# Banded attention by two steps at a time, with one output bank and two banks for turned probabilities

## The reference

```python
scores = scale * np.matmul(q, k.transpose(0, 1, 3, 2))
rel = pos[:, None] - pos[None, :]
is_global = pos[None, :] < int(n_global)            # n_global = 8
is_local = (rel >= 0) & (rel < int(n_local))        # n_local = 96
keep = is_global | is_local
dist = np.where(is_global & ~is_local, float(n_local), np.abs(rel))
scores = scores - slopes[:, None, None] * dist      # slopes by head
scores = np.where(keep, scores, -1e9)
a = softmax(scores); out = np.matmul(a, v)
```

## Time and profile before

| | us |
|---|---|
| median of 3 runs | 1066.98 (1065.27 to 1067.94) |
| profiled execution | 1066.19 |
| its span | 1064.5 |
| PE busy | 944.0 (89%) |
| DVE busy | 691.9 (65%) |
| ACT busy | 443.8 (42%) |
| granted PE clock, mean | 0.923 of full |

### The profile page before, as it was taken

One profiled execution on the slowest core, in us unless ns is written; L12 is line 12 of the kernel. 1 busy time (PEld: TensorE's weight loads), 2 busy tenths in 40 slices (PEclk: granted clock), 3 DMA queues, 4 the chain that ended last, 5 costly groups with the idle time before them and its releaser, 6 DMA issues.

```text
span 1064.5 us, 22298 instructions
## 1 busy us (share of the span) xinstructions
PE 944.0 (89%) x6394; PEld 772.3 (73%) x6397; DVE 691.9 (65%) x1855; ACT 443.8 (42%) x950; POOL 187.8 (18%) x247
## 2 busy tenths in 40 slices
PE   6999999977699999999999993444599999999994
PEld 4667777665488888888888883333388989898984
DVE  5787887758775869878787775555545544464521
ACT  3777777744553534525525251000033434252410
POOL 1222222300111111111111110000113122321211
PEclk8999999989799999999999997555699999999997
DMA  9677676533171515334333342000134444535100
GB/s 212 133 154 143 143 148 147 119 128 143 26 271 39 197 49 197 126 120 178 127 139 119 128 149 97 2 2 2 31 109 155 172 157 169 197 128 195 52 30 30
DMA packets 146569, 129.41 MB, mean 122 GB/s; under 512 B 102464, under 2 KB 114752, under 8 KB 146368
## 3 DMA queue, kind: packets, MB, share of 16 engines
q1 hardware_dynamic: 137696, 99.68, 31.8%
q0 software_dynamic: 8800, 28.84, 8.0%
HBM read 107.79 MB, written 20.71 MB: 121 GB/s over the span
## 4 chain that ended last, share of the span: by engine, by line
PE 78%; DVE 9%; issue 5%; SPq 2%; DVEq 2%; ACT 1%; DMA 1%; ACTq 0%; POOL 0%; POOLq 0%
PE ps_o L1272 14%; PE ps_s L1249 14%; PE ps_o L1614 8%; PE ps_s L1598 6%; PE ps_pT L1598 6%; PE ps_s L1614 4%; PE ps_pT L483 4%; PE ps_o L501 4%; PE ps_s L470 3%; PE ps_t L1775 3%; PE ps_pT L1260 2%; PE ps_t L455 1%; PE ps_o L510 1%; PE ps_t L1235 1%; DVE arena_p L689 1%
## 5 line engine op out<-in xcount | busy, mean ns | idle before, releaser
L1272 PE MATMUL ps_o<-w_split_parts,hs 128*128 x696 | 168.7, 398 | 7.5 <-issue 7.5
L1249 PE MATMUL ps_s<-w_split_parts,xs 128*128 x696 | 165.5, 393 | 1.0 <-ACT xs L1341 1.0
L1272 PEld LDWEIGHTS ps_o<-w_split_parts,hs 128*128 128x128 f32 x696 | 130.0, 190 | 34.9 <-issue 8.0
L1459 DVE SCALAR_TENSOR_TENSOR product<-y_sb,wg_all 128x512 bf16<-128x512 f32 x224 | 145.8, 688 | 10.7 <-issue 5.2
L1249 PEld LDWEIGHTS ps_s<-w_split_parts,xs 128*128 128x128 f32 x696 | 128.6, 188 | 26.6 <-issue 1.3
L1614 PE MATMUL ps_o<-w_split_parts,hs 128*128 128x512 f32 x384 | 94.4, 397 | 0.0
L800 ACT ACTIVATE arena_p<-arena_p,min_s 128x256 f32<-128x256 f32 (+1 forms) x192 | 91.9, 485 | 5.1 <-DVE min_s L678 5.1
L1450 DVE TENSOR_TENSOR w_split_parts<-raw,w_split_parts 128x1024 f32 (+1 forms) x68 | 78.8, 1220 | 19.2 <-ACT w_split_parts L1360 17.8
L1614 PEld LDWEIGHTS ps_o<-w_split_parts,hs 128*128 128x128 f32 x384 | 70.2, 188 | 16.2 <-ACT hs L1648 2.9
L1694 DVE TENSOR_TENSOR w_split_parts<-raw,w_split_parts 128x1024 fp32r<-128x1024 f32 x56 | 68.6, 1224 | 18.3 <-ACT w_split_parts L1656 18.1
L678 DVE CUSTOM_DVE_ANT_0 arena_p<-ps_s,arena_b 128x256 f32<-128x256 f32 (+1 forms) x144 | 53.8, 392 | 39.7 <-PE ps_s L470 16.9
(11 more groups left out here) (307 smaller groups left out, 1653.1 us busy)
## 6 DMA issues: line engine op xcount, KB each, us to landing
raw<-in_moe_w SPq DMA_DIRECT2D x32, 2048.0 KB, 9.1
y_rows<-y_sb POOLq DMA_DIRECT2D x31, 256.0 KB, 2.4
kn<-in_k SPq DMA_DIRECT2D x32, 192.0 KB, 3.5
qn<-in_q SPq DMA_DIRECT2D x32, 192.0 KB, 3.8
vn<-in_v SPq DMA_DIRECT2D x32, 192.0 KB, 3.2
x_rows<-arena_x SPq DMA_DIRECT2D x96, 64.0 KB, 1.6
va<-in_v SPq DMA_DIRECT2D x32, 120.0 KB, 3.1
wg_rows<-in_moe_w_gate SPq DMA_DIRECT2D x1, 2048.0 KB, 8.1
```

The source lines that it names most:

```text
L1249: last = nc.tensor.matmul(ps_s[:, f, :], xs[:, a, c * P:(c + 1) * P], weights(par, w, cols), start=(n == 0), stop=(n == len(passes) - 1))
L1272: last = nc.tensor.matmul(ps_o[:, 0, :], hs[:, a, c * P:(c + 1) * P], weights(par, 2 + w, slice(c * DM, (c + 1) * DM)), start=(n == 0), st ...
L1459: nc.vector.scalar_tensor_tensor(product[:, e % 2, :], y_sb[:], 1.0, wg_all[:, e, :], ALU.mult, ALU.mult, accum_out=log_now[:, e:e + 1])
```

## The change

Steps are taken in twos. `two_pairs` runs over t = 0 to 5, and two-step t has the steps 2t and 2t + 1.
- Scores: both steps of a two-step are scored in one group, into two banks of 512 columns (256 for each step), and the two pairs of banks take turns. The fourth score bank is now `ps_o[:, 1]`, so that `ps_o[:, 0]` is the one output bank; the freed `ps_pT[:, 1]` makes a second bank for turned probabilities.
- Turned probabilities and value products of both steps are issued in groups.
- `copy_cols`, `turn_back` and `norm` run every two steps, over 256 columns; adding and inverting the sums is a function of its own, `invert`.
- Four steps can be held, not three. Steps 3, 7, 9 and 11 are kept by ACT.
- The turns are placed one in each two-step (all three in round 0 of the first pass), and ACT's and DVE's parts of a group stand in the same two-step as the turn; `splits_of` is gone.
- ACT's exps go one two-step ahead of the turned probabilities: in round t it does those of steps 2t + 2 and 2t + 3, which are biased in the same round.
- Counts of semaphores are adapted, in the dense form too, which doesn't run with these inputs.

The core of the diff:

```diff
-        KEPT_BY_ACT = (2, 4, 8, 10)
+        TWOS = QT
+        KEPT_BY_ACT = (3, 7, 9, 11)
         def turns_of(first, last_one):
+            if last_one:
+                return {0: [(0, 2)]}
+            return {0: [(0, 0), (0, 1), (0, 2)] if first else [(0, 2)], 1: [(1, 0)], 2: [(1, 1)], 3: [(1, 2)], 4: [(2, 0)], 5: [(2, 1)]}
...
             def two_pairs(it, first, last_one):          # PE
+                for t in range(TWOS):
+                    if t + 1 < TWOS or not last_one:
+                        score(it, t + 1)
+                    if t >= 2:
+                        turn_back(it, t - 2)
+                    elif not first:
+                        turn_back(it - 1, t - 2 + TWOS)
+                    turn_probs(it, t)
+                    for nth, g in turns_of(first, last_one).get(t, ()):
                         turn(it * 2 + nth + 1, it + (nth + 1) // 2, (nth + 1) % 2, g)
+                    if t >= 1:
+                        value(it, t - 1)
+                    elif not first:
+                        value(it - 1, TWOS - 1)
...
             def value(it, t):
+                pe.wait_ge(normed, it * 6 + t + NORM0)
...
+            def invert(it, t):                           # DVE
+                s = sums_b[:, 4 * t:4 * t + 4]
+                dve.wait_ge(exped, it * 24 + 4 * t + 4 + ATT0)
                 nc.vector.tensor_scalar(s, s, 1e-9, None, ALU.add)
                 dve.drain()
                 nc.vector.reciprocal(s, s)
                 dve.drain()
...
             def two_pairs(it, first, last_one):          # DVE
+                for t in range(TWOS):
+                    before_it, back = (it, t - 2) if t >= 2 else (it - 1, t - 2 + TWOS)
+                    done_one = t >= 2 or not first
+                    if done_one:
+                        invert(before_it, back)
+                    if t + 1 < TWOS or not last_one:
+                        bias_scores(it, 2 * t + 2)
+                    if done_one:
+                        norm(before_it, back)
+                    if t + 1 < TWOS or not last_one:
+                        bias_scores(it, 2 * t + 3)
+                    for s in (2 * t, 2 * t + 1):
+                        if s not in KEPT_BY_ACT:
+                            keep_turned(it, s)
+                    for nth, g in turns_of(first, last_one).get(t, ()):
                         low_qk(it * 2 + nth + 1, (nth + 1) % 2, g)
...
             def two_pairs(it, first, last_one):          # ACT
+                for t in range(TWOS):
+                    if t + 1 < TWOS or not last_one:
+                        exp(it, 2 * t + 2)
+                    for s in (2 * t, 2 * t + 1):
+                        if s in KEPT_BY_ACT:
+                            keep_turned(it, s)
+                    if t + 1 < TWOS or not last_one:
+                        exp(it, 2 * t + 3)
+                    for nth, g in turns_of(first, last_one).get(t, ()):
                         high_qk(it * 2 + nth + 1, (nth + 1) % 2, g)
+                    if t >= 1:
+                        copy_cols(it, t - 1)
+                    elif not first:
+                        copy_cols(it - 1, TWOS - 1)
```

More of the change, by code:

```diff
@@ L456, in turn @@
                 last.then_inc(qk_turned, 1)
[L458 to L466, removed]
-                    for hh in range(2):
[L468 to L488, removed]
-                    pe.wait_ge(v_in[par], it * 96 + 96)
[L491 to L504, removed]
@@ L511, in turn_back @@
+            def turn_back(it, t):
+                pe.wait_ge(o_copied, it * 6 + t + 1)
+                for j in range(2):
+                    last = nc.tensor.transpose(ps_o[:, 0, j * P:(j + 1) * P], o_cols[:, j * P:(j + 1) * P], ident[:])
                 last.then_inc(o_turned, 1)
             def two_pairs(it, first, last_one):
[L514 to L519, removed]
-                    elif not first:
[L521 to L528, removed]
+                for t in range(TWOS):
[3 more added lines that the diff above has]
+                        turn_back(it, t - 2)
+                    elif not first:
+                        turn_back(it - 1, t - 2 + TWOS)
+                    turn_probs(it, t)
+                    for nth, g in turns_of(first, last_one).get(t, ()):
@@ L535, in pe_banded @@
                 turn(0, 0, 0, g)
-            for s in range(AHEAD):
-                score(0, s)
+            score(0, 0)
             two_pairs(0, True, False)
@@ L712, in two_pairs @@
                         low_qk(it * 2 + nth + 1, (nth + 1) % 2, g)
-                    if s % 3 == 2 and s > 2:
-                        norm(it, s // 3 - 1)
-                    elif s == 2 and not first:
-                        norm(it - 1, 3)
                 if last_one:
-                    norm(it, 3)
+                    for t in (TWOS - 2, TWOS - 1):
+                        invert(it, t)
+                        norm(it, t)
             for g in range(3):
                 low_qk(0, 0, g)
-            for s in range(AHEAD):
+            for s in range(2):
@@ L818, in two_pairs, with copy_cols @@
[L818 to L828 removed]
+            def copy_cols(it, t):
+                act.wait_ge(valued, it * 24 + 4 * t + 4 + ATT0)
+                if not (isinstance(it, int) and it == 0 and t == 0):
+                    act.wait_ge(o_turned, it * 6 + t)
+                nc.scalar.activation(o_cols[:], ps_o[:, 0, 0:2 * P], ACT.Copy).then_inc(o_copied, 1)
```

147 lines of the change are left out of this document (79 added, 68 removed).

## The result

| | before | changed |
|---|---|---|
| median of the runs, us | 1067.46 (1065.27 to 1068.86, 4 runs) | 1102.62 (1102.12 to 1103.87, 4 runs) |
| ratio, 95% interval | | 1.0333 [1.0313, 1.0353] |
| span of the profiled execution, us | 1064.5 | 1100.4 |
| mean granted clock | 0.923 | 0.915 |
| one pass of the attention loop, us | 25.5 | 30.9 |

The change makes the kernel 35 us slower, 3.3%. The attention alone ends 36.7 us later (263.26 - 226.53), so next to nothing is lost behind it. The forecast was 1080, slower, with the range 1065 to 1096: the sign and the mechanism are right, the size is not.

A forecast was written before the change was run, and what follows sets the result against it. It took a DVE to ACT to DVE loop each round to bound attention: start 2.4, six passes 165.6, further rounds 22.6 and 19.2 sum to 209.8 against 196.5, +13.3 on 1066.2 us: 1079.5, say 1080; range 1065 to 1096.

The forecast's parts named there:

- which loop decides: Banded attention: a DVE to ACT to DVE loop once a round makes a pass 27.6 us, 2.1 more than before.
- PE, the output bank and the keeps hide in it: Attention rounds: PE's 3.5 us fit in 4.6; one output bank's cost and DVE's keeps are covered by the loop.
- PE alone: TensorE in an attention pass: 26 fewer shape changes by 0.17 us save 4.4, leaving 21.1 us if nothing makes it wait.
- the new norm: DVE's 256-column norm, absent from the trace, priced like the 256-column copy: 0.42 less 0.08 overlap, 0.34 us.
- Base 1.64 + 0.46 + 0.98 + 0.03 = 3.11: Loop length before high and low parts, in us: DVE to second biases, bias to exp, two exps, release of DVE.
- the 0.61 within the 1.64: DVE's add, reciprocal and what stands before the norm: 0.61 us, from 137.03 to 137.64.
- the 0.46: Link from a bias's start on DVE to its exp on ACT: 0.46 us, from 211.85 to 212.31.
- the 0.03: Link from the end of ACT's high_qk to the release of DVE's low_qk: 0.03 us.
- the keep counted as 0.3 more: ACT's 0.48 us keep between exps in rounds 1, 3, 4, 5: second exp at 1.92 against 1.61, so 0.3 more.
- the rival of the clock: PE's idle waits drop its clock to 1.2 GHz one round in three: +34 us, 1113 us; chance 0.07.
- "Faster": Loop not closed, ACT reaches high_qk before DVE reaches low_qk; DVE's 22.0 us bound a pass: 1042 us; chance 0.15.
- The 1036: By the skill's mode-switch rule alone, PE bounds attention at 21.1 us a pass: 31 us less, 1036 us.

The follow-up runs named there:

- the first experiment: The changed kernel with ACT's high_qk moved right behind exp(2t+2), ahead of the keep and exp(2t+3); 1064.44 us, 0.9974 of the kernel before.
- before_unrolled: The kernel before with its six middle passes written out on PE, DVE and ACT instead of looped; 1065.56 us, 0.9989 of the kernel before.
- unrolled: The changed kernel with its six middle passes written out on PE, DVE and ACT instead of looped; 1095.38 us, 1.0275 of the kernel before.
- spread_invert: The changed kernel with high_qk early, PE's turn right behind the score, and sums' add and reciprocal semaphore-ordered, used a round later; 1057.31 us, 0.9912 of the kernel before.

## Why the prediction was right in kind and short in size

- **Right: which loop decides.** "ACT's high_qk now stands behind an exp whose scores DVE biases in this same round, and DVE's low_qk waits for that high_qk." DVE had no idle time before its low parts; now it has in every round of the loop, released by the high part, and moving the high part alone gives everything back (1064.44).
- **Right: PE, the output bank and the keeps hide in it.** Between 100 and 240 us PE waits 20.8 us for the norm, and its loads 22.5 for `o_cols`; still, freeing the bank earlier made the kernel slower. Of the holes one a round is left, the others are covered by waits.
- **Right: PE alone.** Its 21.1 us a pass compare with 21.59 busy in the changed kernel's pass at the full clock and 21.29 in a pass of the first experiment (105.82 to 130.82). Of the 4.4 us that the fewer changes of shape should free, 25.04 - 21.59 = 3.5 came.
- **Right: the new norm.** Estimated at 0.42 us long (0.34 to the next start); rows 130.89 to 131.23 show just that.
- **Failed: the size of a round.** The step that failed is "Base 1.64 + 0.46 + 0.98 + 0.03 = 3.11", of which three terms were too small (the 0.61 within the 1.64, the 0.46 and the 0.03), and with it its rounds. The round shown above was put at 4.62 and took 5.22. The missing 0.60:

| term | forecast | measured | off |
|---|---|---|---|
| add, reciprocal and drains, to the bias | 0.61 | 0.81 | +0.20 |
| bias to exp | 0.46 | 0.61 | +0.15 |
| exp, exp, keep, exp, exp to the high part | 2.44 | 2.47 | +0.03 |
| high part | 0.60 | 0.57 | -0.03 |
| ACT's end to DVE's start | 0.03 | 0.15 | +0.12 |
| the keep counted as 0.3 more, after 0.12 of "address" set against it, which is not on this path | | | +0.13 |

  - The first term was read from a row of the hardware loop (137.03 to 137.64), so the loop is not the main reason that it was too small. What follows the reciprocal is another operation: a norm there, a bias here. With the passes written out on both sides it is 0.50 up to the norm (before_unrolled) and 0.66 up to the bias (unrolled), 0.16 of the 0.20. Why a bias starts later than a norm isn't settled.
  - The second was read where the pass is written out (211.85 to 212.31). There it holds: unrolled shows 0.47, the loop 0.61. This one is the loop's.
  - The third, the 0.03, is about right in another place. Rows of ACT and of DVE of the kernel before show 0.04 from ACT's end at 225.33 to DVE's start, below; the same trace has 0.15 as well (from ACT's end at 817.16 to DVE's start at 817.31), and the low parts take 0.13 to 0.15 in the loop and written out alike. What parts the two values isn't settled.
```profile
224.84 0.49 ACT L816 ACTIVATE o_cols<-ps_o 128x384 f32<-128x384 f32 x1 [2.38 <-PE ps_o L501]
...
225.37 0.17 DVE L695 TENSOR_SCALAR sums<-sums 128x6 f32<-128x6 f32 x1 [0.33 <-ACT o_cols L816]
```

  The other rounds are off by 0.45 to 0.60 likewise, and six of them make the pass 30.9 instead of 27.6.
- **The sum.** 6 x 3.3 = 19.8 of the 23.4 us by which attention ended later than forecast (36.7 against 13.3). The rest: the start +0.6 (the low part of group 0 of pair 2 was done at 33.0, not 32.4), rounds written out of the loop +1.8, the five rounds at the end +1.3 (20.5 against 19.2).
- **The bounds failed with it.** They allowed each released wait "0.03 to 0.10 instead, up to +6", and the link from bias to exp was read at one place, 211.85, which lies in the last pass, written out with constants. What that link costs inside the loop was not asked, though nearly all the rounds are there, nor what follows in the one row from which the add and the reciprocal were priced. The upper end, 1096, lies 6.6 us short.
- **The clock.** "Waits of 1 us should leave it at 2.4 GHz" was wrong. Windows of 2 us of the changed kernel, before and behind an idle time of 1.37 us in front of 139.57:
```profile
138.00:140.00 2.00, 0.83 (x10) 0.63 (x7) 0.60 (x1) 1.52 (x6) 2.00 (x2) 0.85 0.40 118
140.00:142.00 2.00, 2.00 (x12) 2.00 (x11) 1.52 (x10) 0.46 (x3) 0.95 (x1) 0.50 0.48 119
```
  PE, busy 0.83 of 2 us, fell to 0.50, the 1.2 GHz level, and was busy through all of the next 2 us. It did not count: the round from 140.24 to 145.24 shows no wait for PE on the circle, and the pass at the full clock takes 30.87 us as well. So the rival of the clock was right that the level can fall; in the passes of 0.94 the fall cost nothing. Its own condition, one round in three, did not come, and its 34 us stay untested.
- **The rivals.** "Faster" needed ACT to reach the high part before DVE wants it; it did in no round of the changed kernel's loop. With that granted by the first experiment, and the add and the reciprocal taken out, the pass came to 23.2, not the 22.0 of DVE alone that the rival gave; no version run reached its 1042. The 1036 that follows from the switches of tiling mode alone did not come either: the holes went, but PE was not the bound. On the rule itself of the Trainium skill (TensorEngine Tiling (Array Packing), Key Properties: a change of mode drains TensorE) the trace after agrees, with 27 holes of 0.17 us before the score between 100 and 240 us, one a round.

What stays open: neither two halves of one bank nor two whole banks for the output were tried. That the single bank costs nothing under the circle is shown by the norm moved ahead; what it costs in spread_invert, where DVE waits up to 0.8 us for the turn back, is not.

## What to carry to other kernels

When steps are put into groups, write down for each engine's queue what every instruction waits for, and ask whether two engines now wait for each other within one group: the period is then the sum of that circle, however idle each engine is, and moving one instruction ahead of a wait on the same engine can be worth more than the whole change (here 38 us, against the 3 by which the change with its circle open beats the kernel before). Price each link of such a circle from a place where that wait really ends last, in the same kind of loop and with the same instruction behind it. Tiny operations with drains behind them are worth signing off by a semaphore and using a round later where they stand on such a circle: that alone gave 30 us here, and 6 with the circle open (1063.53 to 1057.31).

## What the runs showed of the hardware

- The same steps take longer in a hardware loop than written out with constants: bias to exp 0.61 against 0.47 us, add to bias (with two drains) 0.81 against 0.66, add to norm in the kernel before 0.61 against 0.50. Whether the thresholds of the waits or the addresses cost it, no run tells. On the circle it was 7.2 us of the whole; off it the whole time did not change (before_unrolled, 1065.56), although its passes were 0.5 us shorter.
- From ACT's end to the start of a released DVE instruction it was 0.15 us here (133.85 to 134.00), and 0.04 at 225.33 in the kernel before.
- The granted clock fell to the 1.2 GHz level behind 1.37 us of idle time at 139.57, and stayed at the full one behind the same 1.37 us at 154.97:
```profile
139.57 0.29 PEld L512 LDWEIGHTS ps_o<-ident,o_cols 128*128 128x128 f32 x2 [1.37 <-ACT o_cols L830]
...
154.97 0.20 PEld L512 LDWEIGHTS ps_o<-ident,o_cols 128*128 128x128 f32 x2 [1.37 <-ACT o_cols L830]
```
  The gap alone thus does not tell what the clock will do; the weight load itself shows the level, 0.29 us against 0.20.
